# Softmax reciprocals of an attention and MoE kernel: from VectorE to a power on GpSimd

## What is computed

```python
scores = scale * np.matmul(q, k.transpose(0, 1, 3, 2))
kth = np.partition(scores, -32, axis=-1)[..., -32:-31]
scores = np.where(scores >= kth, scores, -1000000000.0)
scores = scores - np.max(scores, axis=-1, keepdims=True)
attn = np.exp(scores)
attn = attn / (np.sum(attn, axis=-1, keepdims=True) + 1e-09)
x = rows_of(np.matmul(attn, v))              # 2304 x 512
h = x @ w_in
g = np.maximum(h, 0.0) + np.log1p(np.exp(-np.abs(h)))
x = g @ w_out
# then: out[token] = gate * (relu(x @ w1[e]) @ w2[e]), e the argmax of x @ w_gate
```

## Time and profile before

| what | value |
|---|---|
| executions | 1056.10, 1057.04, 1057.84 us |
| median | 1057.04 us |
| the profiled execution | 1057.04 us |
| its span (first to last instruction) | 1054.8 us |
| mean granted TensorE clock | 0.983 of full speed |
| busy: TensorE, VectorE, ScalarE, GpSimd | 94%, 77%, 69%, 67% of the span |

### The profile page before, as it was taken

How to read it: one execution, slowest core, us unless ns; L and a number is a source line. 1 busy time by engine, 2 the same in 40 slices (tenths; PEclk the granted TensorE clock), 3 DMA queues, 4 the chain that set the end, 5 groups by cost and what they waited for, 6 DMA issues and landing times.

```text
span 1054.8 us, 21596 instructions
## 1 busy us (share of the span) xinstructions
PE 992.9 (94%) x6878; PEld 806.3 (76%) x6879; DVE 817.3 (77%) x1744; ACT 727.6 (69%) x1390; POOL 711.9 (67%) x831
## 2 busy tenths in 40 slices
PE   5565899999999999999999999999999999999996
PEld 2343687788788788788788888887887788888875
DVE  7999999999999999999999999994345622222261
ACT  3888898988998998998888999998554111111140
POOL 2688898889899899899888899899351311111101
PEclk9996899999999999999999999999999999999999
DMA  9723253343344343324434333333481421111100
GB/s 311 257 91 127 112 171 121 128 143 121 114 153 165 114 157 121 124 98 144 169 119 155 117 120 102 121 121 121 156 331 54 165 96 52 40 40 40 40 20 20
DMA packets 43391, 130.99 MB, mean 124 GB/s; under 512 B 4320, under 2 KB 18656, under 8 KB 33056
## 3 DMA queue, kind: packets, MB, share of 16 engines
q1 hardware_dynamic: 40256, 120.09, 32.5%
q0 software_dynamic: 3040, 9.70, 2.7%
HBM read 111.95 MB, written 18.09 MB: 123 GB/s over the span
## 4 chain that ended last, share of the span: by engine, by line
PE 80%; DVE 8%; POOL 4%; ACT 3%; issue 3%; DMA 1%; SPq 1%; ACTq 0%; DVEq 0%; POOLq 0%
PE psum L614 8%; PE psum L575 7%; PE psum L644 7%; PE psum L737 6%; PE psum L739 6%; PE psum L738 6%; PE psum L646 6%; PE psum L645 6%; PE psum L663 6%; PE psum L665 6%; PE psum L664 6%; PE psum L589 5%; DVE top L1158 3%; DVE work L1164 3%; PE psum L769 2%
## 5 line engine op out<-in xcount | busy, mean ns | idle before, releaser
L1158 DVE MAX8 top<-work 128x8 f32<-128x576 f32 x432 | 305.4, 752 | 0.0
L1164 DVE MATCH_REPLACE8 work<-top,work 128x576 f32<-128x576 f32 x288 | 212.6, 749 | 0.0
L644 PE MATMUL psum<-x_parts,wi_hi 128*128 128x256 f32 x576 | 171.1, 297 | 0.0
L645 PE MATMUL psum<-x_parts,wi_hi 128*128 128x256 f32 x576 | 162.9, 283 | 0.0
L646 PE MATMUL psum<-x_parts,wi_lo 128*128 128x256 f32 x576 | 162.7, 283 | 0.0
L614 PE MATMUL psum<-prT,vtok 128*64 128x128 f32 (+3 forms) x1600 | 117.1, 287 | 15.2 <-ACT prT L918 15.2
L614 PEld LDWEIGHTS psum<-prT,vtok 128*64 128x64 f32 (+1 forms) x1600 | 85.5, 144 | 54.2 <-issue 41.2
L575 PE MATMUL psum<-kT,qT 64*128 64x512 f32 (+3 forms) x640 | 113.0, 480 | 11.5 <-DMA qT<-in_q 4.4
L1638 POOL DMA_INDIRECT out<-ys,dst_now x19 | 19.2, 1012 | 152.6 <-DVE ys L1360 150.7
L663 PE MATMUL psum<-wo_ring,h_hi 128*128 x288 | 119.1, 414 | 1.0 <-POOL h_lo L1547 0.9
L1541 POOL TENSOR_TENSOR hs<-hs,ab 128x512 f32<-128x512 f32 x72 | 93.7, 1301 | 32.7 <-ACT ab L941 32.5
(11 more groups left out here) (215 smaller groups left out, 2353.1 us busy)
## 6 DMA issues: line engine op xcount, KB each, us to landing
wo_ring<-wo_parts SPq DMA_DIRECT2D x72, 1024.0 KB, 4.8
wo_parts<-wo_ring SPq DMA_DIRECT2D x8, 1024.0 KB, 3.8
kT<-in_k SPq DMA_DIRECT2D x16, 288.0 KB, 3.4
qT<-in_q SPq DMA_DIRECT2D x16, 288.0 KB, 3.9
vtok<-in_v SPq DMA_DIRECT2D x16, 256.0 KB, 2.9
wo_raw<-in_moe_w_out SPq DMA_DIRECT2D x1, 4096.0 KB, 14.1
wi_raw<-in_moe_w_in SPq DMA_DIRECT2D x4, 1024.0 KB, 14.4
x_rows<-x2tok SPq DMA_DIRECT2D x16, 256.0 KB, 2.4
```

What stands on the lines that cost most here:

```text
L644: nc.tensor.matmul(ps[:, part, :], wi_hi[:, u, kk, f], hi, start=first, stop=False)
L645: nc.tensor.matmul(ps[:, part, :], wi_hi[:, u, kk, f], lo, start=False, stop=False)
L1158: nc.vector.max(top[:, at, 8 * r:8 * r + 8], sc_of(n)[:, t, :] if r == 0 else work[:, t, :]).then_inc(topk_step, 1)
L1164: nc.vector.match_replace(work[:, t, :], top[:, at, 8 * r - 8:8 * r], sc_of(n)[:, t, :] if r == 1 else work[:, t, :], TAKEN).then_inc(topk ...
```

## The change

GpSimd gets a constant tile `inverse` of minus ones. From block 9 on, `denominators` waits for its own addition and raises the sum to the power of minus one, which gives `rden`. VectorE's `reciprocals` is called for blocks 0 to 8 alone, so its condition goes away, and so do its calls in the top-k loop and behind it. The wait that keeps the two-deep `den` and `rden` from being written over changes: it now asks that both tiles of block n - 2 have been normalised (`pr_ready`), where before it asked for the reciprocal of block n - 2.

```diff
+        inverse = sb("inverse", [P, 2])
...
+        inverse_ready = sem("inverse_ready")
...
             def reciprocals(n):
-                if n < MLP_AT - 1:
-                    dve.wait_ge(exp_ready, 2 * n + 2)
-                    nc.vector.tensor_reduce(den[:, n % 2, :], eps[:, n % 2], AX.X, ALU.add
-                                            ).then_inc(den_step, 1)
+                dve.wait_ge(exp_ready, 2 * n + 2)
+                nc.vector.tensor_reduce(den[:, n % 2, :], eps[:, n % 2], AX.X, ALU.add
+                                        ).then_inc(den_step, 1)
                 dve.wait_ge(den_step, n + 1)
                 nc.vector.reciprocal(rden[:, n % 2, :], den[:, n % 2, :]).then_inc(rden_ready, 1)
...
-                    if r == 1 and n > MLP_AT:
-                        reciprocals(n - 2)
                     for t in range(2):
                         maxima(n, t, r)
                 if 0 < n < MLP_AT:
                     reciprocals(n - 1)
-            reciprocals(BLOCKS - 2)
-            reciprocals(BLOCKS - 1)
...
             def denominators(n):
                 pool.wait_ge(exp_ready, 2 * n + 2)
                 if n >= 2:
-                    pool.wait_ge(rden_ready, n - 1)
+                    pool.wait_ge(pr_ready, 2 * n - 2)
                 nc.gpsimd.tensor_tensor(den[:, n % 2, :], eps[:, n % 2, :, 0], eps[:, n % 2, :, 1],
                                         ALU.add).then_inc(den_step, 1)
+                pool.wait_ge(den_step, n + 1)
+                nc.gpsimd.tensor_tensor(rden[:, n % 2, :], den[:, n % 2, :], inverse[:], ALU.pow
+                                        ).then_inc(rden_ready, 1)
...
             nc.gpsimd.memset(eps[:], 1e-9).then_inc(consts, 1)
+            nc.gpsimd.memset(inverse[:], -1.0).then_inc(inverse_ready, 1)
...
+            pool.wait_ge(inverse_ready, 1)
             for i in range(TAIL):
```

## The result

The changed kernel takes 1067.58 us (median of 4 runs, 1066.54 to 1068.31); the kernel before takes 1056.89 us (median of 4). The ratio is 1.010, with a 95% interval of 1.0083 to 1.0118: the change costs 10.7 us. The forecast was 1059.8 us, in a range of 1056.4 to 1078. The profiled execution took 1068.31 us; its span is 11.8 us longer than before.

A forecast was written before the change was run, and what follows sets the result against it. TensorE was taken to bound the main stage, with GpSimd nearly full. Runs of equal cycles +1.4, first cycles +0.2 and last cycles +1.2 made 2.8 us on 1057.04: 1059.8 us, range 1056.4 to 1078.

The forecast's parts named there:

- What bounds the kernel now: Section on the stage from 120 to 700 us: TensorE sets the pace, VectorE 98.9% and GpSimd 91.3% busy.
- rival B: GpSimd becomes the bound from a power of 0.62 us; every further 0.1 us costs 5.8 us; chance 0.17.
- the forecast case: Power of 0.45 to 0.65 us on GpSimd, mostly absorbed by its waits; 1059 to 1066 us; chance 0.40.
- I take 0.5 us: Assumed length of the 128x2 power on GpSimd, between bounds of 193 ns and 1430 ns.
- A cycle grows by the power less 0.1 us: Each GpSimd cycle with a power becomes longer by 0.4 us, for a power of 0.5 us.
- The slack of the stage: GpSimd's waits for ScalarE from 140 to 720 us, 30.4 us or 0.52 a step, absorb 23 us more work.
- The stalls in runs of three equal cycles: In six runs of three 9.45 us GpSimd cycles, lag reaches 1.2 us, 0.24 too much for TensorE: +1.4 us.
- the start: First cycles after 120 us: one or two lags gather before the first long cycle, +0.2 us.
- The last cycles: Last cycles before 735 us, where GpSimd is the chain: three lags, +1.2 us.
- the cover: Lag the path from softplus through ScalarE to TensorE's normalised block can take before TensorE waits: 0.96 us.
- VectorE's 10.5 and 21.6 us valued at nothing: VectorE loses 63 reciprocals, 10.5 us busy, and 21.6 us of waits for den; no gain, as no engine waits for it.
- Rival C: VectorE, 98.9% busy, was the hidden bound; freeing its queue gains 1 to 2 us, 1055.5 us; chance 0.06.

The follow-up runs named there:

- experiment 4: The changed kernel with ten extra instructions on GpSimd at its start, powers and sums of 1 to 16 elements, each waited for; 1067.43 us.
- experiment 7: The changed kernel without the add of den: GpSimd raises the sum of the exponentials itself to minus one; 1057.12 us, ratio 1.0009.
- experiments 5 and 6: The kernel before plus a product behind GpSimd's add of den: an unread short one of 0.20 us, 1055.32 us; one of 96 elements, 1055.94 us.
- Experiment 1: The kernel before plus the power on GpSimd into a tile nobody reads, reciprocals still on VectorE; 1067.18 us, ratio 1.0106.

## Why the prediction was right or wrong

**The direction and the place were right.** "What bounds the kernel now" called GpSimd nearly full with equal cycles of 9.45 us, and rival B gave the mechanism. What happened is B and not the forecast case. B had a chance of 0.17 and the forecast case 0.40, whose own range ended at 1066; the time lies in the full range because that took in the lower half of B. That the time fell inside the range is in part luck.

**The term that failed is the length of the power.** The step "I take 0.5 us" should have had 0.72. Its per-element part, 0.14 us from an assumed hundred operations, came close to the 0.157 us of experiment 4 by luck, as no row stood behind the hundred; the fixed part failed: it was taken from the small sum (0.19 us) and is 0.39 us. With 0.72 in rival B's own line the prediction would have read 58 x (0.62 - 0.52) = 5.8 us and 3 to 4 at both ends, 1066 to 1067 us, against 1067.58.

**A cycle grows by the power less 0.1 us:** right in kind. 0.62 us was due and 0.65 was measured; for the product of 0.20 us, 0.10 was due and 0.09 to 0.12 measured.

**The slack of the stage** was 30.4 us, 0.52 a cycle. The added 62 x 0.65 = 40.3 us cost 12.2, so 28.1 were absorbed. This reading of the waits was the one that carried the result.

**The stalls in runs of three equal cycles** did not come. In experiment 7, with a growth of 0.36 us, they, the start and the last cycles were to cost 2.4 us; it cost 0.7, and TensorE waited 0.3 us in place of 1.1 for the normalised block. The forecast's 2.8 us rested on the runs and the start for more than half. At a growth of 0.4 us the kernel would, by an estimate from experiment 7, have stood at about +0.7 us, no change: the forecast case had the wrong number for its own power. Part of it is a miscount. The three starts of den at 407.86, 417.31 and 426.75 us bound two cycles of 9.45 us; three powers do fall between two waits of GpSimd there (one ends at 398.68 us, the next at 435.01), but between 140 and 720 us there are four such stretches, not six, which makes 1.0 us of the 1.4. Whether the cover is larger than 0.96 us is open, since the lag in experiment 7 reached only 1.0.

**The last cycles** (three lags, 1.2 us) are there: in experiment 7, with a growth of 0.36 us, the last 14 cycles take 1.6 us more than before. That its whole time is only 0.7 us longer goes with the 319.1 us behind the last of them, 1.0 us less than before. But experiments 5 and 6, with hardly a lag, have the same there, so this is not a cost of the power given back. Where the 1.0 us comes from is open.

**VectorE's 10.5 and 21.6 us valued at nothing:** right. Experiment 1 keeps them and takes the same time as the changed kernel to 0.4 us. Rival C falls with it.

**The new wait for pr_ready valued at nothing:** right, by the same experiment, which has the old wait.

**The rule on the choice of engine** (the Trainium skill, GPSIMD Engine Reference, "Engine selection": additions, products and maxima of two inputs are about 2x slower on GpSimd than on VectorE) gave an estimated 0.33 us. Measured are 0.72 us for the power on GpSimd and 0.166 us for the reciprocal on VectorE, 4.3x: its direction holds here, its factor is not that of a power, which it doesn't list.

**What would show it** named the case: "Wrong by B: GpSimd without any wait, TensorE with gaps in every cycle." GpSimd's waits are 0.4 us; TensorE's gaps are gathered, 6.1 us of them before the first unit of a group, where it asks for x_parts, a path that the prediction had not priced.

## What to carry to other kernels

An engine that works through a fixed list each step has a hard floor: the length of the list. Sum the waits of such an engine for others over the stage; here that sum, 30.4 us, was about all that could be added to it (28.1 us), and beyond it each instruction is paid in full, in every step, whether or not anyone reads its result. Before moving a small instruction, measure the one on the new engine by itself: the rare operation, not the neighbour of the same size, sets the price. And in a full list put it ahead of a wait, where it fills time, and spread it rather than bunch it.

## What the runs showed of the hardware that was not expected

A power on GpSimd has a fixed cost of its own, 0.39 us against 0.19 for a sum of the same shape, and then 0.157 us an element of each partition (16 elements: 2.90 us; a sum of 16: 0.22). Exponent 3 costs the same as minus one. And the second of two powers, which need not wait, adds 0.60 us to a cycle in which GpSimd never waits, where the first with its wait for den adds 0.65.
